# A routed two-layer kernel: the last tile's scores on TensorE, bids of 40 tiles made earlier, weight pieces issued together

## The reference

```python
# x: the first mixture's output, 4608 rows of 512; E = 8, F = 1024, cap = 576
logits = x @ w_gate
order = np.argsort(-logits.flatten())
for idx in order:                       # best pair (token, expert) first
    tok, e = idx // E, idx % E
    if assigned[tok] >= 0 or counts[e] >= cap:
        continue
    assigned[tok] = e
    counts[e] += 1
    ...
for e in range(E):
    mask = assigned == e
    h = np.maximum(x[mask] @ w1[e], 0.0)
    out[mask] = h @ w2[e]
```

## Time and profile before

| | us |
|---|---|
| median of three runs | 1503.86 |
| the profiled execution | 1500.03 |
| its span, first to last instruction | 1498.2 |

### The profile page before, as it was taken

One profiled execution on the slowest core, in us unless ns is written; L12 is line 12 of the kernel. 1 busy time (PEld: TensorE's weight loads), 2 busy tenths in 40 slices (PEclk: granted clock), 3 DMA queues, 4 the chain that ended last, 5 costly groups with the idle time before them and its releaser, 6 DMA issues.

```text
span 1498.2 us, 26945 instructions
## 1 busy us (share of the span) xinstructions
PE 1315.6 (88%) x9724; PEld 1084.6 (72%) x9724; DVE 974.1 (65%) x2214; ACT 441.3 (29%) x784; POOL 397.5 (27%) x324
## 2 busy tenths in 40 slices
PE   5988718898999999999993169999999999999997
PEld 5877616786888888888882157878777777787885
DVE  1566793677567677776667768585758585767420
ACT  1655522122222222222220032423232323233431
POOL 1244426747616172480000001111111111111110
PEclk9989858999999999999996569999999999999999
DMA  9999128694514143241100304040404132222310
GB/s 218 253 271 289 57 45 297 220 352 154 156 43 155 42 157 106 89 146 49 43 22 15 124 18 148 30 152 30 145 30 132 50 117 65 82 93 84 104 32 18
DMA packets 71168, 173.48 MB, mean 116 GB/s; under 512 B 11624, under 2 KB 30136, under 8 KB 70400
## 3 DMA queue, kind: packets, MB, share of 16 engines
q1 hardware_dynamic: 46576, 108.61, 24.8%
q0 software_dynamic: 12368, 40.92, 8.6%
q10 hardware_dynamic: 12096, 22.19, 4.7%
HBM read 130.47 MB, written 41.23 MB: 115 GB/s over the span
## 4 chain that ended last, share of the span: by engine, by line
PE 67%; DVE 16%; DMA 6%; issue 5%; POOL 5%; ACT 1%; SPq 0%; DVEq 0%; POOLq 0%; ACTq 0%
PE bank L687 50%; PE bank L775 5%; PE bank L730 4%; POOL w_lo L524 3%; PE o_ps L648 2%; DMA xst<-x_rows,tok_i 2%; DMA x_sorted<-xst 1%; DMA v_sb<-in_v 1%; PE kv_ps L614 1%; POOL w_hi L522 1%; DMA w_sb<-in_moe_w 1%; PE bank L723 1%; PE bank L716 1%; DVE xrow L1052 1%; PE qt_ps L636 1%
## 5 line engine op out<-in xcount | busy, mean ns | idle before, releaser
L1202 DVE SCALAR_TENSOR_TENSOR bank<-bank,factor,wg2b 128x512 f32<-128x512 f32 x344 | 260.6, 758 | 10.8
L1189 DVE TENSOR_TENSOR hT_lo<-bank,hT_hi 128x512 fp32r<-128x512 f32 x166 | 107.0, 685 | 194.0 <-ACT hT_hi L932 185.0
L899 ACT ACTIVATE h<-bank 128x512 f32<-128x512 f32 x166 | 99.2, 598 | 356.8 <-PE bank L687 335.7
L687 PE MATMUL bank<-w_hi,xT_hi 128*128 (+1 forms) x664 | 193.1, 413 | 10.7 <-POOL w_lo L524 6.4
L687 PE MATMUL bank<-w_lo,xT_hi 128*128 (+1 forms) x664 | 190.6, 403 | 0.4 <-DVE w_lo L1237 0.4
L687 PE MATMUL bank<-w_hi,hT_hi 128*128 (+1 forms) x664 | 180.8, 411 | 6.2 <-DVE score L1205 3.3
L687 PE MATMUL bank<-w_hi,xT_lo 128*128 (+1 forms) x664 | 182.9, 397 | 0.0
L578 POOL DMA_INDIRECT xg<-y_rows,gat_i x40 | 41.6, 1040 | 502.3 <-DVE sca_i L1376 283.1
L687 PE MATMUL bank<-w_lo,hT_hi 128*128 (+1 forms) x664 | 173.4, 402 | 0.0
L687 PE MATMUL bank<-w_hi,hT_lo 128*128 (+1 forms) x664 | 171.0, 398 | 0.0
L687 PEld LDWEIGHTS bank<-w_hi,xT_lo 128*128 128x128 f32 x664 | 125.6, 189 | 30.5 <-issue 0.2
(11 more groups left out here) (238 smaller groups left out, 1803.1 us busy)
## 6 DMA issues: line engine op xcount, KB each, us to landing
w_sb<-in_moe_w SPq DMA_DIRECT2D x112, 512.0 KB, 5.0
y_rows<-y ACTq DMA_DIRECT2D x43, 256.0 KB
x_sorted<-xst SPq DMA_DIRECT2D x41, 260.0 KB
xg<-x_sorted ACTq DMA_DIRECT2D x41, 260.0 KB
k_sb<-in_k SPq DMA_DIRECT2D x16, 576.0 KB, 15.5
v_sb<-in_v SPq DMA_DIRECT2D x16, 576.0 KB, 17.3
q_sb<-in_q SPq DMA_DIRECT2D x8, 1152.0 KB, 20.6
x_rows<-xrow POOLq DMA_DIRECT2D x16, 576.0 KB, 6.3
```

What stands on the lines that cost most here:

```text
L687: mm = pe.matmul(ps, a[:, i % chunks, :], b[:, i % chunks, cols], start=(i == 0), stop=(i == 3 * chunks - 1))
L899: act.activation(h[:, half * HALF:(half + 1) * HALF], h_ps[half][:, :], ACT.Relu).then_inc(s_h, 1)
L1189: dve.tensor_tensor(hT_lo[:, half * 4:(half + 1) * 4, :].rearrange("p a b -> p (a b)"), th_ps[half][:, :], hT_hi[:, half * 4:(half + 1) * ...
L1202: ch.link(dve.scalar_tensor_tensor(out=prod_ps[:, :], in0=y1_ps[t % 2][:, :], scalar=factor[:, t:t + 1], in1=wg2b[:, e, :], op0=ALU.mult, ...
```

## The change

- The scores of the last tile (42) leave VectorE. TensorE transposes the scaled rows `ys[0]` into `tx_ps`, ScalarE copies them into `h`, TensorE multiplies them with the gate `wg2_sb` into eight columns of `th_ps[0]`, and VectorE takes the minimum with `cap_v` into `score`. VectorE's loop over the tiles is one iteration shorter.
- The bids and the first comparison are made for tiles 0 to 39 in the iteration `t = 41` of VectorE's first loop, and for the last 3 tiles at the start of selection 0. The payload's digits, the room and its negative move into the iteration `t = 39`.
- `a3`, `cmp`, `posf` and `lst` lie where `segment` and `onehot` were; other small buffers change their order.
- The first selection copies `taken` in place of clearing it and adding.
- SP issues the eight pieces of a load one behind the other and waits only for all of them.
- `select(0, 0)` is counted apart from `select(1, 1)`, whose number of chained operations the loop uses.

```diff
 # SP, load_phase
                 for i in range(PIECES):
                     w, at = (w21, i) if i < PIECES // 2 else (w22, i - PIECES // 2)
-                    wait_pos(sp, s_wp[i % 2], (kk * (PIECES // 2) + i // 2) * 16)
-                    alone(sp)
                     sp.dma_start(w_sb[:, u, i * w_piece:(i + 1) * w_piece],
...
 # TensorE, behind the loop over the tiles
+            pe.wait_ge(s_y, T1)
+            for c in range(KC):
+                mm = pe.transpose(tx_ps[:, c * P:(c + 1) * P], ys[(T1 - 1) % 2][:, c * P:(c + 1) * P], ident[:, :])
+            mm.then_inc(s_yt, 1)
+            pe.wait_ge(s_ytc, 1)
+            for c in range(KC):
+                mm = pe.matmul(th_ps[0][:, 0:E], h[:, c * P:(c + 1) * P], wg2_sb[:, c, :], start=(c == 0), stop=(c == KC - 1))
+            mm.then_inc(s_ysc, 1)
...
 # ScalarE, behind its loop
+            act.wait_ge(s_yt, 1)
+            act.activation(h[:, 0:DM], tx_ps[:, :], ACT.Copy).then_inc(s_ytc, 1)
             weights_high(0, 0, range(PIECES // 2 + 2))
...
 # VectorE
+            def bid_on(gs):
+                n = gs.stop - gs.start
+                full = [P, n, E]
+                link(dve.tensor_reduce(best[:, gs], score[:, gs, :], AX, ALU.max))
+                ch.inc(dve.tensor_scalar(m43[:, 1, gs], best[:, gs], -INPLAY, 100.0, ALU.is_lt, ALU.mult))
+                link(dve.tensor_tensor(a3[:, gs, :], score[:, gs, :], best[:, gs].unsqueeze(2).to_broadcast(full), ALU.is_equal))
+                link(dve.tensor_tensor(a3[:, gs, :], a3[:, gs, :], rank8[:, :].unsqueeze(1).to_broadcast(full), ALU.mult))
+                link(dve.tensor_reduce(m43[:, 0, gs], a3[:, gs, :], AX, ALU.max))
+                link(dve.tensor_tensor(m43[:, 0, gs], m43[:, 0, gs], m43[:, 1, gs], ALU.add))
+                link(dve.tensor_tensor(bid[:, gs, 0:E], a3[:, gs, :], m43[:, 0, gs].unsqueeze(2).to_broadcast(full), ALU.is_equal))
...
+            known = slice(0, T1 - 3)
+            rest = slice(T1 - 3, T1)
...
-            for t in range(T1 + 2):
+            for t in range(T1 + 1):
                 if t > 2:
                     scores(t - 2)
...
+                if t == T1 - 4:
+                    link(dve.tensor_scalar(pos_i[:, 0, :], tok_i[:, :], 6, None, ALU.logical_shift_right))
...
+                    link(dve.memset(room[:, :], float(CAP)))
+                    less_room()
+                if t == T1 - 2:
+                    dve.wait_ge(s_sc, T1 - 3)
+                    dve.wait_ge(s_clear, 1)
+                    bid_on(known)
+                    ch.inc(compare(known, thr0[:, 0, :]))
+            dve.wait_ge(s_ysc, 1)
+            dve.wait_ge(s_sc, T1 - 1)
+            link(dve.tensor_scalar(score[:, T1 - 1, :], th_ps[0][:, 0:E], cap_v[:, T1 - 1:T1], None, ALU.min))
...
 # VectorE, select
+                first = isinstance(kk, int) and kk == 0
+                every = slice(0, T1)
+                if first:
+                    bid_on(rest)
+                else:
+                    less_room()
+                    bid_on(every)
                 for r in range(R):
                     thr = thr_i[:, :] if r else thr0[:, 0, :]
+                    ask(compare(rest if first and r == 0 else every, thr))
...
+                if first:
+                    link(dve.tensor_copy(taken[:, :, :], a3[:, :, :]))
+                else:
+                    link(dve.tensor_tensor(taken[:, :, :], taken[:, :, :], a3[:, :, :], ALU.add))
```

More of the change, by code:

```diff
@@ L140, in build @@
         rank8 = sb("rank8", [P, E])
-        segment = sb("segment", [PT, E, G1])
+        with ExitStack() as ranks:
+            segment = ranks.enter_context(nc.sbuf_tensor("segment", [PT, E, G1], F32))
+            onehot = ranks.enter_context(nc.sbuf_tensor("onehot", [PT, E, G1], F32))
+        a3 = sb("a3", [P, T1, E])
+        cmp = sb("cmp", [P, T1, NTH], F16)
+        posf = sb("posf", [P, 2, T1])
+        lst = sb("lst", [P, T2, 4])
         digits = sb("digits", [P, R, NTH], I32)
@@ L155, in build @@
         sc_raw = sb("sc_raw", [P, E])
-        onehot = sb("onehot", [PT, E, G1])
         tok_i = sb("tok_i", [P, T1], I32)
@@ L234, in build @@
         s_sc = sem("scores_done")
+        s_yt = sem("last_y_turned")
+        s_ytc = sem("last_y_copied")
+        s_ysc = sem("last_scores")
         s_sel = sem("select_dve")
@@ L336, in build @@
         ohb = sb("ohb", [P, T1, P], F16)
-        cmp = sb("cmp", [P, T1, NTH], F16)
-        a3 = sb("a3", [P, T1, E])
         b3 = sb("b3", [P, T1, E])
         taken = sb("taken", [P, T1, E])
+        oha2 = sb("oha2", [P, T1, T2], F16)
+        ra2 = sb("ra2", [P, T1, T2, 4], F16)
+        tn = sb("tn", [P, NTH])
+        sums = sb("sums", [P, 2, E])
+        tots = sb("tots", [P, 3, E])
+        e8 = sb("e8", [P, 4, E])
+        n_i = sb("n_i", [P, R], I32)
+        base_i = sb("base_i", [P, 2], I32)
+        low_i = sb("low_i", [P, R], I32)
+        thr_i = sb("thr_i", [P, NTH], I32)
+        sums_h = sb("sums_h", [P, 2, E], F16)
+        sc1 = sb("sc1", [P, 8])
         room_n = sb("room_n", [P, P], F16)
@@ L344, in build @@
         m43 = sb("m43", [P, 4, T1])
[L345 to L352, removed]
         room = sb("room", [P, E])
-        e8 = sb("e8", [P, 4, E])
-        sc1 = sb("sc1", [P, 8])
         mtot_h = sb("mtot_h", [P, 1], F16)
         pos_i = sb("pos_i", [P, 3, T1], I32)
[L358 to L361, removed]
         block = ctx.enter_context(nc.Block())
@@ L923, in y_copy @@
                     act.wait_ge(s_yst[w], (T1 + 1 - w) // 2 * 16)
-                    act.wait_ge(s_sc, T1)
+                    act.wait_ge(s_sc, T1 - 1)
                 else:
@@ L1205, in scores, with compare, less_room @@
                 dve.tensor_scalar(score[:, t, :], sc_raw[:, :], cap_v[:, t:t + 1], None, ALU.min).then_inc(s_sc, 1)
+            def bid_on(gs):
[8 more added lines that the diff above has]
+                link(dve.tensor_tensor(bid[:, gs, 0:E], a3[:, gs, :], m43[:, 0, gs].unsqueeze(2).to_broadcast(full), ALU.is_equal))
+            def compare(gs, thr):
+                full = [P, gs.stop - gs.start, NTH]
+                return dve.tensor_tensor(cmp[:, gs, :], best[:, gs].unsqueeze(2).to_broadcast(full),
+                                         thr.bitcast(F32).unsqueeze(1).to_broadcast(full), ALU.is_ge)
+            def less_room():
+                ch.inc(dve.tensor_scalar(room_n[0:1, 0:E], room[0:1, :], -1.0, None, ALU.mult))
+            known = slice(0, T1 - 3)
+            rest = slice(T1 - 3, T1)
             factor_kept(0)
@@ L1220, in _ @@
                     scores(0)
[L1223 to L1231, removed]
+                if t == T1 - 4:
+                    link(dve.tensor_scalar(pos_i[:, 0, :], tok_i[:, :], 6, None, ALU.logical_shift_right))
+                    ch.inc(dve.tensor_scalar(pos_i[:, 1, :], tok_i[:, :], 63, None, ALU.bitwise_and))
+                    ch.inc(dve.tensor_copy(payload2[:, :, 2], pos_i[:, 0, :]))
+                    ch.wait()
+                    link(dve.tensor_copy(payload2[:, :, 3], pos_i[:, 1, :]))
+                    link(dve.memset(room[:, :], float(CAP)))
[8 more added lines that the diff above has]
+            link(dve.tensor_scalar(score[:, T1 - 1, :], th_ps[0][:, 0:E], cap_v[:, T1 - 1:T1], None, ALU.min))
             def weights_low(kk, u, i):
@@ L1283, in select @@
                 bids = bid[:, :, 0:E]
[L1285 to L1296, removed]
+                first = isinstance(kk, int) and kk == 0
[5 more added lines that the diff above has]
+                    bid_on(every)
                 for r in range(R):
                     thr = thr_i[:, :] if r else thr0[:, 0, :]
-                    ask(dve.tensor_tensor(cmp[:, :, :], best[:, :].unsqueeze(2).to_broadcast([P, T1, NTH]),
-                                          thr.bitcast(F32).unsqueeze(1).to_broadcast([P, T1, NTH]), ALU.is_ge))
+                    ask(compare(rest if first and r == 0 else every, thr))
                     ask(dve.tensor_scalar(ind[:, :], cps[:, 0:NTH], 0.0, None, ALU.is_ge))
@@ L1350, in select @@
                 link(dve.tensor_tensor(a3[:, :, :], a3[:, :, :], b3[:, :, :], ALU.add))
-                link(dve.tensor_tensor(taken[:, :, :], taken[:, :, :], a3[:, :, :], ALU.add))
+                if first:
+                    link(dve.tensor_copy(taken[:, :, :], a3[:, :, :]))
+                else:
+                    link(dve.tensor_tensor(taken[:, :, :], taken[:, :, :], a3[:, :, :], ALU.add))
                 link(dve.tensor_tensor(b3[:, :, :], taken[:, :, :], over_g(es), ALU.mult))
@@ L1383, in select @@
                 link(dve.tensor_tensor(score[:, :, :], score[:, :, :], over_g(t8), ALU.min))
+            select(0, 0)
             start = ch.n + ch.base
-            select(0, 0)
+            select(1, 1)
             per = ch.n + ch.base - start
-            select(1, 1)
             with dve.Fori(1, E // 2) as j:
-                ch.enter(j * (2 * per) + start)
```

(1 more changed line is left out.)

## The result

The changed kernel takes 1491.45 us (median of 6 runs, 1487.95 to 1495.6) against 1503.94 (6 runs, 1502.26 to 1506.2): ratio 0.9916, 95% interval 0.9898 to 0.9934. Run again beside its variants it took 1491.03 (12 runs, 1487.1 to 1498.04) against 1499.7 (33 runs, 1494.1 to 1508.4): 0.9939, 0.9918 to 0.9961. The two agree only near the ends of their intervals, and single executions of one kernel lie up to 14 us apart. So I read the terms from traces, stage by stage, and use the times for the sum. The profiled execution took 1490.97 with a span of 1489.2; before it was 1500.03 and 1498.2.

The account below looks back on a forecast made before the run. TensorE was taken to bound the mixtures and a dependent chain, mostly on VectorE, the stretch between; 9.3 from the chain plus 0.5 at the loop's turns took 9.8 us off 1503.86, giving 1494.1, range 1488.5 to 1498.

Parts of the forecast that it names:

- What bounds the stretch: Between the mixtures: one chain of dependent steps, mostly on VectorE, sets the time; only what leaves it counts.
- Scores on TensorE: Last tile's scores by transposes, copy, small matmuls and minimum, from 793.44 to 796.85 instead of VectorE until 802.3.
- Bids: Before the first search: only 3 tiles' bids remain, 1.3 us plus 0.25; first count at 798.4, 9.2 us earlier.
- The copy of `taken`: First selection: a copy replaces an addition of 128x344; 0.1 us taken off.
- The cover inside the mixture: Iteration of tile 41: 3.7 us of early bids delay scores(40) but cost nothing, with 0.1 and 0.7 us to spare.
- Rival 2: First mixture's end: moved bids are late and TensorE waits, costing 1.2 to about 3 us (1497); chance 0.04, shared.
- The loads: Weight pieces all in flight: a load takes 14 to 16 us instead of 21, but nobody waits, so nothing comes off.
- the 0.5 us that I gave to the loop's turns: VectorE's two loop turns in the second mixture: less load contention saves a quarter microsecond each.
- Rival 1: VectorE's loop turns lose their stall and the half clock after it: 6.7 us in all, 1487.9; chance 0.10.
- Rival 3: Second mixture: gathers queue behind eight weight pieces, 21 us lost over seven phases, 1515; chance 0.04.
- Rival 4: Weight loads: the deeper queue moves nothing faster, loads stay at 21 us; 1494.6, inside the forecast's 0.78.
- The sum: Whole kernel: 9.3 from the chain plus 0.5 from the loop's turns, 9.8 us off.

Follow-up runs that it names:

- e3: The kernel before with only the last tile's scores moved to TensorE, bids of all 43 tiles still made at once after them: 1493.32 us, ratio 0.9962.
- e4: The changed kernel with the last tile's scores back on VectorE, early bids and loads as changed: 1498.54 us, ratio 0.998.
- e5: The changed kernel with the seven bid operations on 40 tiles made twice in a row: 1495.44 us, ratio 0.9963.
- e6: The changed kernel with VectorE's loop over pairs of phases written out, so that no branch is taken: 1483.84 us, ratio 0.989.
- e1: The changed kernel with SP's weight pieces paced as before, two in flight: 1492.61 us, ratio 0.9949.
- e2: The kernel before with all eight weight pieces in flight and nothing else changed: ratio 0.9986.
- a0: The changed kernel run again unaltered, beside its variants: 1491.03 us, ratio 0.9939.

## Why the prediction was right, and where it was not

- **What bounds the stretch.** Right: 9.1 us came off the chain and the two stages behind it moved along unchanged (67.6 for 67.8, 622.5 for 622.8).
- **Scores on TensorE.** Forecast 3.4 from ScalarE's start to the ready minimum (793.44 to 796.85), measured 3.4 (793.96 to 797.36). Each piece was sized from the nearest row: transposes 0.67 for 0.66, copy 0.61 for 0.60, products 1.07 for 1.05, VectorE's wait 1.44 for "some 1.4". Eight columns were no cheaper than thirty-two.
- **Bids.** From the minimum's end to the first count 1.55 forecast, 1.6 measured (seven operations at 0.1 to 0.2, comparison 0.22). The chain gave 9.1 where 9.2 was forecast; the bids and the scores each moved by what their rows said, as e3 and e4 show apart (6.1 and 3.6, 0.6 of it shared). The copy of `taken` took 0.35 in place of 0.53: 0.18, with 0.1 forecast.
- **The cover inside the mixture.** Right: scores(40) ended 0.8 before the product started, forecast 0.7, and TensorE's wait stayed 1.48. The sum left out the hand-over of 0.27, so the cover was thinner than forecast, 0.6; e5 shows the edge and that half clock comes on top. Rival 2 was the right mechanism beyond it: e5 lost 3.9 us where 2.4 went over the cover.
- **The loads.** Right that nobody waits, and in the length (13.1 to 15.4 from the first issue to the last packet, forecast 14 to 16). Wrong in the 0.5 us that I gave to the loop's turns. The failed step is the reading that the turn stands "in the tail of the load": only the first 0.7 of the 3.71 us did, and with the load over VectorE stood 4.10 and 3.76 us, for 3.96 and 3.37 before. The term is 0.
- **Rival 1** was real as a mechanism and wrong as a result: the stall costs what I priced (6.7; e6 shows 5.3 and 8.7 without and with the spells, 1.5 of it away from the turns), but the change doesn't touch it. **Rival 3** didn't happen: TensorE waits for no gathered row, and the loads end 2 to 4 us before the first gather of their phase is issued (1067.0 and 1069.56 for one). **Rival 4** is refuted, the loads are a third shorter.
- **The sum.** 9.3 by the traces for 9.8: the time came out in the range with a term of 0.5 in it that is nothing. The four stages of the table add up to 9.8 less, but 0.5 of that lies in the two mixtures, where executions of one kernel differ by more; it is chance, and not the forecast's 0.5. The spans lie 9.0 apart, as the first product started 0.8 later. The measured medians lie 12.5 apart in the first comparison and 9.1 by the ratio of the second. I don't explain the 3 us between them by the change: e1 and e2 exclude the loads by their traces, and the start of the first product alone lay anywhere from 230.8 to 236.7 us in the ten profiles (232.1 and 236.4 in the two of the changed kernel), in stages whose instructions no kernel here alters. What makes those stages vary was not tried.

## What to carry to other kernels

Where two engines hand each other steps, size each moved step by the nearest row of its shape and end the sum at the engine that arrives last; that gave 9.2 for 9.1. A buffer's reader, not only its engine's idle time, limits what can be slipped into a loop: here 3.8 us of idle time before the last low half held 3.7 us of bids, and the next writer of the bank that the scores read had only 0.6 to spare. Filling the DMA queue made loads a third shorter and the kernel no faster, while two holes of 3 to 4 us with nothing issued at a loop's turns, which looked like a load's fault, were worth 4 to 7 us, and writing the loop out 5 to 9. When an experiment takes something out, count in the trace what else went with it.

## What the runs showed that I had not expected

- Two turns of VectorE's loop, whose body is two selections, stalled it 7.3 (before) and 7.4 us (e1) together, with the last 0.5 to 1.2 us of a load beside each, and 7.9 (after), 7.0 (a0) and 7.9 us (e2) with no load. ScalarE's turn of its own loop at 1180.9 cost 0.04, SyncE's at 1067.5 0.14. Between two branches the trace of the changed kernel has 485 recorded instructions on VectorE, 131 on ScalarE and 62 on SyncE.
- A gap of about 2 us on TensorE is followed by 3.4 us at 1.2 GHz in some executions and not in others of the same kernel: behind 2.34 and 1.99 us in the first profile of the changed kernel, not behind 1.76 and 1.71 in the second. It is mostly the longer gaps, but 1.57 in the kernel before had a spell and 2.16 in e1 had none. Two such spells make some 2.7 us of the second mixture.
- The DMA engines moved 342 and 408 GB/s in four-microsecond stretches with eight pieces of 512 KB queued, and 206 to 256 in five such stretches of the first load with two.
